# Where VectorE makes its weight sums between two layers, and an accumulator on its small operations

## The reference, cut to what matters

```python
scores = (q @ k.T) / sqrt(64); scores = cap * tanh(scores / cap)      # 2 batches, 12 heads, 448 rows, 64 wide
attn = exp(scores - max) / (sum + 1e-9); x = (attn @ v) as (896, 768)
h = x @ w_in;  g = where(h > 0, h, exp(min(h, 0)) - 1); x = g @ w_out  # 768 -> 2048 -> 768
h = x @ w_in2; g = maximum(0.01 * h, h);               y = g @ w_out2  # the same sizes
```

## Time and profile before

| | |
|---|---|
| median of 3 runs | 581.84 us (581.84 to 583.5) |
| the profiled execution's own time | 582.32 us |
| its span, first to last instruction | 580.5 us |
| TensorE busy | 560.0 us, 96% |
| VectorE, ScalarE, GpSimd busy | 479.3, 353.4, 281.2 us |
| granted TensorE clock, mean | 0.997 of full speed |

### The profile page before, as it was taken

One profiled execution on the slowest core, in us unless ns is written; L12 is line 12 of the kernel. 1 busy time (PEld: TensorE's weight loads), 2 busy tenths in 40 slices (PEclk: granted clock), 3 DMA queues, 4 the chain that ended last, 5 costly groups with the idle time before them and its releaser, 6 DMA issues. The chain is left out here.

```text
span 580.5 us, 8583 instructions
## 1 busy us (share of the span) xinstructions
PE 560.0 (96%) x2908; PEld 501.3 (86%) x2908; DVE 479.3 (83%) x731; ACT 353.4 (61%) x606; POOL 281.2 (48%) x273
## 2 busy tenths in 40 slices
PE   7999879999999999999999999989999999999997
PEld 6676758888998999999999999879999998899996
DVE  5899999989887223897999998789999788999871
ACT  5999978999996455654644455445454455544440
POOL 5879998799976656552000002586666520000000
PEclk8999999999999999999999999999999999999999
DMA  6354545445432233335644432031113225536251
GB/s 174 93 150 124 124 127 155 129 123 138 114 86 70 92 110 108 110 108 165 217 137 146 153 85 80 1 109 55 55 55 91 74 82 191 162 111 217 83 169 49
DMA packets 34172, 67.07 MB, mean 116 GB/s; under 512 B 6864, under 2 KB 18768, under 8 KB 34128
## 3 DMA queue, kind: packets, MB, share of 16 engines
q1 hardware_dynamic: 33984, 66.28, 38.9%
q10 hardware_dynamic: 144, 0.23, 0.1%
HBM read 63.70 MB, written 2.80 MB: 115 GB/s over the span
## 5 line engine op out<-in xcount | busy, mean ns | idle before, releaser
L557 POOL TENSOR_TENSOR w_lo<-w_raw,w_hi 128x768 fp32r<-128x768 f32 (+1 forms) x62 | 105.7, 1707 | 55.5 <-ACT w_hi L619 54.9
L557 POOL TENSOR_TENSOR w_lo<-s_sum,w_hi 128x384 fp32r<-128x384 f32 x32 | 37.8, 1195 | 119.1 <-ACT w_hi L619 119.1
L619 ACT ACTIVATE w_hi<-s_sum 128x768 fp32r<-128x768 f32 (+1 forms) x64 | 43.4, 684 | 78.7 <-DVE s_sum L876 54.5
L619 ACT ACTIVATE w_hi<-w_raw 128x768 fp32r<-128x768 f32 (+1 forms) x77 | 56.5, 737 | 31.6 <-PE o_ps L1118 16.0
L599 ACT ACTIVATE soft<-soft,neg_max 112x448 f32<-112x448 f32 x96 | 63.3, 666 | 4.9 <-DVE soft L755 4.8
L755 DVE TENSOR_SCALAR_CACHE_REDUCE soft<-soft,neg_abs 112x448 f32<-112x448 f32 x96 | 60.7, 669 | 2.6 <-ACT soft L589 2.2
L1116 PE MATMUL mlp_ps<-x_hi,w_hi 128*128 128x448 f32 x132 | 49.2, 373 | 0.4 <-issue 0.4
L1117 PE MATMUL mlp_ps<-x_lo,w_hi 128*128 128x448 f32 x132 | 48.2, 365 | 0.0
L1118 PE MATMUL mlp_ps<-x_hi,w_lo 128*128 128x448 f32 x132 | 48.2, 365 | 0.0
L589 ACT ACTIVATE soft<-scores 112x896 f32<-112x896 f32 x47 | 43.1, 918 | 6.8 <-PE scores L1077 6.7
L762 DVE TENSOR_TENSOR p_lo<-probs_t,p_hi 112x896 fp32r<-112x896 f32 x37 | 40.2, 1087 | 6.3 <-ACT p_hi L608 6.2
(11 more groups left out here) (236 smaller groups left out, 1751.5 us busy)
## 6 DMA issues: line engine op xcount, KB each, us to landing
w_raw<-w_units SPq DMA_DIRECT2D x120, 384.0 KB, 3.1
q_raw<-qT SPq DMA_DIRECT2D x24, 224.0 KB, 2.9
k_raw<-kT SPq DMA_DIRECT2D x23, 224.0 KB, 2.8
v_raw<-v_rows SPq DMA_DIRECT2D x24, 112.0 KB, 2.9
inv_all<-inv_rows SPq DMA_DIRECT2D x24, 112.0 KB, 3.1
y_t<-y_out SPq DMA_DIRECT2D x12, 224.0 KB, 2.9
inv_rows<-row_inv SPq DMA_DIRECT2D x24, 1.8 KB, 2.9
k_raw<-kT ACTq DMA_DIRECT2D x1, 224.0 KB, 3.2
```

What stands on the lines that cost most here:

```text
L557: pool.tensor_tensor(w_part(w_lo, n), w_source(n), f32(w_part(w_hi, n)), ALU.subtract).then_inc(w_lo_pool, 1)
L619: nc.scalar.activation(w_part(w_hi, n), w_source(n), ACT.Copy).then_inc(w_hi_done, 1)
```

## The change

Three edits, all on VectorE's and ScalarE's order or operations.

1. Two operations get an accumulator output that nothing reads (`unread`): the 24 additions of 1e-9 to the row sums in `invert`, and the three roundings of `w_high` on VectorE.
2. The border of the layers. The four weight sums of block 1, which stood together behind `add_to(0, "p4")`, are made earlier: two ahead of `x_low("p1")`, one behind the first `x_sum`, one behind the second. ScalarE rounds y21 (`x_high("p2")`) behind four roundings of weights and `block_keep(0)` rather than ahead of them. VectorE takes `x_low("p2")` ahead of the `block_add`s, and the results of (0,p3) and (0,p7) ahead of the difference for p4.
3. In the second layer's output one weight sum, that of item 5, goes from ahead of item 4's work to behind it.

```diff
@@ ScalarE
             x_high("p6")
-            x_high("p2")
             w_high(GEMM1 + 6)
             w_high(GEMM1 + 7)
             for q in range(GEMM1 + 1, GEMM2[1]):
                 if p == "p1" and i != 1:
                     block_keep(i)
+                if i == 0 and p == "p1":
+                    x_high("p2")
@@ VectorE
-                nc.vector.tensor_scalar(row_den[:, h % 2, :], row_sum[:, h % 2, :], EPS, 1.0, ALU.add, ALU.mult
-                                        ).then_inc(den_done, 1)
+                nc.vector.tensor_scalar(row_den[:, h % 2, :], row_sum[:, h % 2, :], EPS, 0.0, ALU.add, ALU.add,
+                                        accum_out=unread[0:QT, h % 2:h % 2 + 1]).then_inc(den_done, 1)
...
-                nc.vector.tensor_copy(w_part(w_hi, n), w_source(n)).then_inc(w_hi_dve, 1)
+                nc.vector.tensor_scalar(w_part(w_hi, n), w_source(n), 1.0, 0.0, ALU.mult, ALU.add, accum_out=unread[:, 2 + n:3 + n]
+                                        ).then_inc(w_hi_dve, 1)
...
+                    late = l == 1 and n == PQ
+                    if n + 1 < FULL2 and GEMM2[l] + n + 1 in SUM_ITEMS and not late:
                         weight_sum(GEMM2[l] + n + 1)
...
                     g_low(l, n)
+                    if late:
+                        weight_sum(GEMM2[l] + n + 1)
...
+            weight_sum(GEMM1 + BLOCK_AT[1, "p5"])
+            weight_sum(GEMM1 + BLOCK_AT[1, "p6"])
             x_low("p1")
             x_sum(y12, y12, y11, ALU.subtract)
+            weight_sum(GEMM1 + BLOCK_AT[1, "p3"])
             x_low("p5")
             x_sum(y11, y22, y11, ALU.add)
+            weight_sum(GEMM1 + BLOCK_AT[1, "p7"])
             x_low("p6")
             add_to(0, "p4", y21, kept_u2[0], y21_done)
-            for p in SUMS:
-                weight_sum(GEMM1 + BLOCK_AT[1, p])
+                if i == 0 and p == "p6":
+                    x_low("p2")
                 if p == "p6":
                     block_add(i, "p6")
                 if i == 0 and p == "p6":
                     block_add(0, "p3")
-                    x_low("p2")
+                    block_add(0, "p7")
                     block_hidden(0, "p3")
-                    block_add(0, "p7")
+                    block_hidden(0, "p7")
                     x_sum(y21, y21, y11, ALU.subtract)
-                    block_hidden(0, "p7")
```

More of the change, by code:

```diff
@@ L181, in build @@
         neg_abs, cap_inv, s_scale = sb("neg_abs", [P, 1]), sb("cap_inv", [P, 1]), sb("s_scale", [P, 1])
+        unread = sb("unread", [P, 2 + AHEAD])
         neg_max = sb("neg_max", [QT, 2, 2])
@@ L912, in second @@
                         add_to(l, "p2", y[2], kept_p1[l], y11_done)
-                    if n + 1 < FULL2 and GEMM2[l] + n + 1 in SUM_ITEMS:
+                    late = l == 1 and n == PQ
+                    if n + 1 < FULL2 and GEMM2[l] + n + 1 in SUM_ITEMS and not late:
                         weight_sum(GEMM2[l] + n + 1)
```

## The result

| | before | after |
|---|---|---|
| median, runs side by side | 582.21 us (581.84 to 583.5) | 576.14 us (575.31 to 577.16) |
| ratio | | 0.9893, 95% interval 0.9869 to 0.9916 |
| the profiled execution's own time, and its span | 582.32, 580.5 us | 575.31, 573.5 us |
| VectorE, GpSimd busy | 479.3, 281.2 us | 472.1, 277.5 us |
| granted TensorE clock, mean | 0.997 | 0.997 |

The kernel became 1.1% faster; 576.0 was forecast. The two profiled executions lie 7.0 us apart, and I place these one after the other.

What follows compares the result with a forecast made beforehand. TensorE, busy 96% of the span, bounds the kernel outside three places with idle time. Attention 2.9, border 1.5 and item 5's sum 1.4 take 5.8 us off 582.32: 576.5, median 576.0; range 572.8 to 579.8.

Steps and rivals of the forecast that it cites:

- Additions: In `invert`, each addition with the accumulator takes 0.16 us plus a read of 0.08, 0.24 us, without waiting for GpSimd.
- Attention: From 42 to 112 us, VectorE's freed waits give TensorE 2.9 us, with 0 and 5.5 as ends.
- GpSimd's relief: In attention, GpSimd gains beside the roundings: an `x_lo` there took about 1.2 us more than a `q_stack` of the same length.
- The stall further on: Beyond the attention's first stretches, a TensorE stall of 1.1 us that goes too only at the 5.5 us end.
- Roundings: On VectorE in attention, each of three roundings takes 1.08 us with its read, 3.2 in all: 0.1 us lost.
- The estimate by the Trainium skill: Three roundings cost about 0.4 us each more on VectorE, taking at most 1.2 us off the attention's gain.
- Border: At the border of the layers, TensorE's waits shrink by 1.5 us; ends 1.3 of loss and 2.4 of gain.
- the collision for p2's rest: At the border, p2's rest finds GpSimd's last `w_lo` running, starts at 377.4 and ends at 378.8 us.
- Item 5's sum: In `second(1)`, moving the sum behind item 4's work gains 1.4 us; ends 0.8 and 1.6.
- attention nothing or all: Two rivals: attention gives nothing, 578.9 us, chance 0.15; attention gives 5.5 and the border 2.4, 572.5 us, chance 0.10.
- the slower case: In attention, the roundings' accumulator form holds GpSimd up longer and TensorE waits: 3.4 us slower, 585.2 us, chance 0.05.
- Collisions at the border: Rival: more turns behind GpSimd make p6's and p2's rests 1.5 us later, 577.5 us, chance 0.10.

Runs made afterwards that it cites:

- e2_den: Before with the accumulator on the 24 additions alone, the three roundings unchanged: 579.7 us, ratio 0.9987 to before.
- e5_round: Before with the accumulator on the three roundings alone, the additions unchanged: 585.64 us against 580.87, ratio 1.0091.
- e9_xsum: e6_fill with the difference y21 - y11 ahead of (0,p7)'s result and item 2's `g_last` ahead of the blocks' last result: 574.42 us, ratio 0.9881 to before.
- e4_item5: Before with only the weight sum of item 5 moved behind item 4's work: 581.51 us, ratio 0.9995 to before.
- e6_fill: After with the additions of (0,p6) and (0,p3) ahead of p2's rest, (0,p3)'s result directly behind it: 575.58 us against before's 580.87, ratio 0.9912.
- e7_spread: e6_fill with three of block 1's weight sums one place later and item 2's `g_last` ahead of the blocks' last result: 576.89 us, ratio 0.9932 to before.
- e8_noadd: After without the 24 additions of 1e-9, the reciprocal reading the row sums: 575.97 us, ratio 0.9915 to before.
- e11_after: After unchanged, run once more on another chip: 576.35 us against before's 581.51, ratio 0.9903.

## Why the prediction was right

- **Additions, 0.24 us each**: 0.15 + 0.08 = 0.23. That the form does not wait for GpSimd was read from the 96 maxima, and it holds.
- **Attention, 2.9 us**: 3.05. The size is right, its working only half, and that the sum came out is luck. I priced the additions' waits at 2.9 us of TensorE's time, let the roundings lose VectorE 0.1, and put GpSimd's relief, which I had named, at nothing in the sum. e2_den has 1.5 us for the additions; the other 1.5 came with the roundings, and e5_round shows that they would lose 5 us without the additions' form. Where the time went was right: TensorE's idle time of 42 to 90 us fell by the 2.4 that were said, and from 90 us on VectorE's saving went idle. The stall further on stayed (1.09 us).
- **Roundings, 1.08 us**: 0.93 + 0.07 = 1.00. The estimate by the Trainium skill ("VectorE: DVE Perf Modes", the tier table), 0.4 us more for each on VectorE, is too high for what the traces have: 0.93 against the 0.78 of the fastest copies (before, e2_den), 0.15 more, or 0.22 with the read. Whether even those copies waited for GpSimd is not shown. Against before's mean of 1.03 nothing was lost. The estimate left out what happens on GpSimd meanwhile, and there the sign turns: behind the additions' form, the roundings' slower one is worth 1.5 us.
- **Border, 1.5 us**: 1.2. The steps up to p2's rest came within a tenth of a microsecond, p2's rest itself within 0.3. In before's time p1's rest was to end at 362.9 (359.79 + 3.05 = 362.84), p6's at 373.4 (373.33), the last addition into y21 at 375.0 (374.92), with p2's rest ending at 378.8 (378.55); TensorE lost 0.2 at p6, where 0.3 was said. That VectorE and GpSimd take turns, as the Trainium skill has it ("SBUF — State Buffer", Who interferes with whom), shows at 356.33 (1.16 us for a sum of 0.55).
- **The step that failed** is the end of that part, "The y21 difference and p4's rest end at about 387.4, before (0,p4) wants them at 388". The difference met one more `w_lo` (379.67 beside 379.75) and took 2.35 us, the rest ended at 385.06 + 3.05 = 388.1, and (0,p4) wanted it 0.3 us earlier, since the wait for (0,p7) had gone. I had counted the collision for p2's rest and not for the next long operation of the same chain. That is the 0.3 us between 1.5 and 1.2.
- **Item 5's sum, 1.4 us**: 1.41, and what was said to be next showed up as next in e9_xsum. It is made up otherwise than said, though. Matmul by matmul TensorE won 1.27 us at item 4 and 0.13 behind it, where 1.2 and up to 0.4 were forecast less a stall at the reload. Items 3.65 us apart did not come: VectorE goes on at 3.75 and 3.74 for items 5 to 7. And item 5's `g_last` had 0.3 us to spare (it ends at 485.83 and TensorE takes it at 486.10), not 0.6.
- **The rivals**: attention nothing or all, and the slower case, are excluded by the 3.05 us and the lead of 3.4 us at head 12. Collisions at the border exist, but cost 0.3 us more than said, not 1.5. The slower case's mechanism, a GpSimd and a VectorE that hold each other up until TensorE waits, does exist in this kernel, in the half that I had not thought of (e5_round).
- **The sum**: 5.8 us predicted, 5.65 by the trace (3.05 + 1.19 + 1.41). That the median, 576.14, met the 576.0 so closely is luck as well, at a range of 575.31 to 577.16 in four runs. The 7.0 between the profiled executions, and the 6.07 between the medians, hold in addition how many slow stretches fell on either side.

## What to carry to other kernels

Where two engines hold each other up over SBUF, try the form of an instruction that is slower alone: judge it by the end of the chain and not by its duration, and change all the instructions concerned together, since half of such a change can cost what the whole brings. When a wait of the critical engine is removed, follow the next chain on its new, earlier schedule with every collision of the old one still in it; here 1.2 us won at one wait came back as 1.1 us at the next until the chain itself was shortened. Edits worth 0.2% are told by the waits of a trace, placed edit by edit, when the scatter of the runs is larger than they are.

## What the hardware showed that I had not expected

- Stretches of 50 to 100 us in which matmuls of one shape follow each other every 0.2067 us instead of 0.2027, with a granted clock of 1.00 in the same rows. They cost up to 3.3 us per execution and are found in before, e4_item5, e6_fill, e7_spread, e8_noadd and e11_after. What causes them stays open.
- An addition on four elements lasts up to 2.77 us beside GpSimd (e5_round), and 0.15 with an accumulator output that nothing reads (after).
- A wait of 2.08 us on TensorE in a dense stretch was followed by 3 us at a granted clock of 0.50, and one of 2.76 us at 66 us by a second such fall (e5_round), so that 2 us of lateness cost more than 2 us.
- Attention with the same code took 163.2 to 164.2 us from the first addition to the last in six traces, and 166.3 in all three with the old additions and roundings.
